# Products of values and scores written as two column tiles of 64 tokens

## Chip, cores and metric

The kernel runs on one core of one Trainium2 chip. The metric is the device time of one execution in microseconds (us); lower is better. Of the kernel before there are three timed executions and one profiled execution.

## What is computed

Three layers in a row: a linear recurrence with a decaying state per head, a feed-forward layer of width 2048 with a clipped square as its nonlinearity, and a gated feed-forward layer of width 1536. In the reference, cut to what matters here:

```python
batch, n_heads, seq, head_dim = (4, 8, 768, 48)          # all float32
for t in range(S):                                        # recurrence
    cur = np.einsum('bhd,bhe->bhde', u[None] * kt, vt)
    y[:, :, t] = np.einsum('bhd,bhde->bhe', rt, state + cur)
    state = wt[:, :, :, None] * state + np.einsum('bhd,bhe->bhde', kt, vt)
x = y as 3072 tokens x 384
h = x @ w_in;  g = where(h >= 1, h, where(h <= -1, 0, (h + 1)**2 / 4));  x = g @ w_out
g = x @ w_gate; x = (g * sigmoid(g) * (x @ w_val)) @ w_out
```

## The kernel before

The 3072 tokens are worked on in 8 "halves" g of 384 tokens, and each half in 3 windows w of 128 tokens. A channel-major operand lies with one head on partitions 0 to 47 and the other head of a pair on 64 to 111, so there are 4 pairs of heads.

The recurrence is done in windowed form. For each window TensorE does a list of "fills", each into a PSUM bank that VectorE or ScalarE then empties ("drains"):

- KT (L1082): 4 transposes of the scaled keys.
- AT, two fills in one (L1089): the scores of keys against receptances, a matmul with 48 rows for each head. The two heads of a pair lie on partitions 0 to 47 and 64 to 111. VectorE copies the part above the diagonal into the SBUF tiles `att0` and `att1`, 4 heads each (L894).
- ST (L1098): 4 products of the key transposes (128 x 112) with 96 columns of values: what the window adds to the state.
- Y: the output of the window, 128 tokens (partitions) x 384 channels, one bank. First, unless the state is still zero, 4 matmuls of the receptances with the decayed state (L1104, 128 tokens on the stationary side, 96 moving columns). Then, for each of the 8 heads, one matmul that adds the scores times the values (L1108): stationary operand `att[h % 2][:, h // 2, :]`, 128 x 128; moving operand 48 columns of `vn`. VectorE adds the diagonal term (L908), which gives `x_by_token`.
- XT (L1113): 3 transposes of `x_by_token`, from which ScalarE and VectorE make the high and low parts of x (L681, L911).

These products are plain fp32. For each the trace holds two LDWEIGHTS and two MATMUL records; such a pair of one LDWEIGHTS and one MATMUL is called a record pair below. So L1108 has 16 in a Y fill and 384 in all, in 24 Y fills. The large products of the feed-forward layers (L1039 for the way in, L1063 for the way out) are written as three fp32r products of high and low parts, each with a 128 x 128 stationary operand and 384 moving columns, and leave one record pair each.

The order is written out by hand. The fills of half 0 stand at the head of the program, before the first feed-forward product; that head also loads and splits the weights of layer 1. After that `phase1` runs 8 halves of 16 slots. A slot j has on TensorE the 9 products of `tile_in` (j + 2), then the fills of the next half that `WIN_SLOTS` gives to the slot, then the 9 products of `tile_out` (j):

```python
    FILLS = [("KT", 0, 0), ("AT", 0, 0), ("AT", 0, 1), ("ST", 0, 0), ("KT", 1, 0), ("Y", 0, 0),
             ("AT", 1, 0), ("AT", 1, 1), ("XT", 0, 0), ("ST", 1, 0), ("KT", 2, 0), ("Y", 1, 0),
             ("AT", 2, 0), ("AT", 2, 1), ("XT", 1, 0), ("ST", 2, 0), ("Y", 2, 0), ("XT", 2, 0)]
    WIN_SLOTS = {3 + i: (2 * i, 2 * i + 1) for i in range(NF // 2)}
    WIN_SLOTS[11], WIN_SLOTS[12] = (NF - 2,), (NF - 1,)
```

So the Y fills of halves 1 to 7, 21 of them, stand in slots 5, 8 and 11 of the half before, each between other matmuls of TensorE. `phase2`, the gated layer, has no fills. TensorE takes its instructions in program order; waits on semaphores guard the banks (`bank_free`) and the operands: a Y fill waits for the decayed state (`st_dec`) and for both score tiles (`at_out`), and its last matmul increments `fill`, for which the drain L908 waits.

Of the kernel before, what the change touches and what calls it, by code (L numbers as in the profile page):

```python
# [31 lines left out]
B, H, S, D = 4, 8, 768, 48  # L32
# [3 lines left out]
WIN = 128  # L36
# [47 lines left out]
def build_program(nc, w_d, kd_d, rd_d, rn_d, kn_d, vn_d, u_d, cst_d, w1i_d, w1o_d, w2g_d, w2v_d,  # L84
                  w2o_d, rs_d, ks_d, vs_d, ws_d, us_d, out_d, x2_d, ys_d):
    ctx = ExitStack()
    with ctx:
        at = [nc.sbuf_base + (-nc.sbuf_base) % 32]

        def place(name, shape, dt, offset=None):  # L90

            size = 2 if dt == mybir.dt.bfloat16 else 4
            for n in shape[1:]:
                size *= n
            if offset is None:
                offset = at[0]
                at[0] += (size + 31) // 32 * 32
            assert offset + size <= nc.sbuf_usable_end, (name, offset + size)
            return nc.alloc_sbuf_tensor_at(name, shape, dt, offset=offset), offset + size
# [36 lines left out]
        vn, _ = place("v_by_token", [P, NW, DM], F32)  # L136
        uu, _ = place("u_rows", [P, DM], F32)
        att = [place(f"att{i}", [P, 4, WIN], F32)[0] for i in range(2)]
# [14 lines left out]
        for n in ("hi", "lo"):  # L153
            t, o = place(f"w2gv_a{n}", [P, NA, 2, KT * P], F32R, o)
# [3 lines left out]
        for n in ("hi", "lo"):  # L158
            t, o = place(f"w2gv_b{n}", [P, J2 - NA, 2, KT * P], F32R, o)
            w2b.append(t)  # L160
        w2o = []
        for n in ("hi", "lo"):
            t, o = place(f"w2o{n}", [P, J2, DM], F32R, o)
# [55 lines left out]
        def state_pairs(w, parity):  # L219

            return 1 if parity == 1 and w == NW - 1 else NPAIR
# [26 lines left out]
        def bank_of(g, f):  # L248

            return (attb + hid + acc)[f % 8] if isinstance(g, int) and g == 0 else attb[f % NBANK]  # L250

        def cols(w):
            return slice(w * WIN, (w + 1) * WIN)
# [776 lines left out]
        def _(e):  # L1030
# [36 lines left out]
            def do_fill(g, f, parity):  # L1067
                kind, w, n = FILLS[f]
                if kind == "AT" and n == 1:
                    return  # L1070
                out = bank_of(g, f)
                bank_free(g, f)
                if kind == "KT":
                    first_half = isinstance(g, int) and g == 0
                    if w == 0 and not first_half:
                        e.wait_ge(scaled, (g + 1) * (2 * NPAIR))
                    if w == 0 and isinstance(g, int) and g == 0:
                        e.wait_ge(ld["cst"], 16)
                    for p in range(NPAIR):
                        if w == 0 and first_half:  # L1080
                            e.wait_ge(scaled, 2 * p + 2)
                        m = e.transpose(out[:, p * PR:(p + 1) * PR], kd[:, p, cols(w)], ident[0:PR, 0:PR])  # L1082
                elif kind == "AT":
                    other = bank_of(g, f + 1)
                    bank_free(g, f + 1)
                    for p in range(NPAIR):
                        for i, o in enumerate((out, other)):
                            r = slice(64 * i, 64 * i + D)
                            m = e.matmul(o[:, p * WIN:(p + 1) * WIN], kd[r, p, cols(w)], rd[r, p, cols(w)],  # L1089
                                         start=True, stop=True)  # L1090
                            if p == NPAIR - 1 and i == 0:
                                m.then_inc(fill, 1)
                elif kind == "ST":
                    e.wait_ge(kt_out, g * NW + (w + 1))
                    if w == 0:
                        e.wait_ge(ld["vn"], (g + 1) * 16)
                    for p in range(state_pairs(w, parity)):
                        m = e.matmul(out[0:PR, p * 2 * D:(p + 1) * 2 * D], ktk[w % 2][:, p * PR:(p + 1) * PR],  # L1098
                                     vn[:, w, p * 2 * D:(p + 1) * 2 * D], start=True, stop=True)
                elif kind == "Y":  # L1100
                    e.wait_ge(st_dec, g * NW + (w + 1))
                    row_start = w == 0 and parity == 0
                    for p in range(0 if row_start else NPAIR):
                        e.matmul(out[:, p * 2 * D:(p + 1) * 2 * D], rd[:, p, cols(w)], sbar[:, p, :],  # L1104
                                 start=(p == 0), stop=False, skip_group_check=True)
                    e.wait_ge(at_out, g * (2 * NW) + (2 * w + 2))
                    for h in range(H):
                        m = e.matmul(out[:, h * D:(h + 1) * D], att[h % 2][:, h // 2, :], vn[:, w, h * D:(h + 1) * D],  # L1108
                                     start=(row_start and h == 0), stop=(h == H - 1), skip_group_check=True)
                elif kind == "XT":  # L1110
                    e.wait_ge(y_out, g * NW + (w + 1))
                    for k in range(KT):
                        m = e.transpose(out[:, k * P:(k + 1) * P], xn[:, w, k * P:(k + 1) * P], ident)  # L1113
                m.then_inc(fill, 1)

            def bank_free(g, f):

                n_bank = 8 if isinstance(g, int) and g == 0 else NBANK
                gg, ff = (g, f - n_bank) if f >= n_bank else (g - 1, f - n_bank + NF)
                if isinstance(gg, int) and gg < 0:  # L1120
                    return
                kind, w, n = FILLS[ff]
                if kind == "KT":
                    e.wait_ge(kt_out, gg * NW + (w + 1))
                elif kind == "AT":
                    e.wait_ge(at_out, gg * (2 * NW) + (2 * w + n + 1))
                elif kind == "ST":
                    e.wait_ge(st_out, gg * (2 * NW) + (2 * w + 2))
                elif kind == "Y":
                    e.wait_ge(y_out, gg * NW + (w + 1))  # L1130
                else:
                    e.wait_ge(xl_out, gg * NW + (w + 1))
# [3 lines left out]
            for f in range(NF):  # L1136
                do_fill(0, f, 0)
# [19 lines left out]
            def slot(g, j, parity, next_half, after_next):  # L1157
                last = isinstance(g, int) and g == NG - 1
                if j + 2 < J1:
                    tile_in(g, j + 2, parity)  # L1160
                elif not last:
                    tile_in(g + 1, j + 2 - J1, 1 - parity)
                else:
                    tile_in2(0, j + 2 - J1, 0)
                if last and j == 4:
                    e.wait_ge(w_sum, NG + 2)
                    e.matmul(attb[2][0:1, 0:1], bad[:, OPS_CHECK:OPS_CHECK + 1], ones[:, :], start=True, stop=True).then_inc(w_tot, 1)
                if next_half:
                    for f in WIN_SLOTS.get(j, ()):
                        do_fill(g + 1, f, 1 - parity)  # L1170
                tile_out(1, g, j, w1o)
# [76 lines left out]
```

## Time and profile before

| | us |
|---|---|
| median of 3 executions | 1050.95 |
| lowest, highest | 1050.66, 1052.82 |
| profiled execution, its own time | 1050.49 |
| its span, first to last instruction | 1048.6 |
| TensorE matmuls busy | 1004.0 (96%) |
| TensorE weight loads busy | 990.1 (94%) |
| VectorE busy | 555.8 (53%) |
| ScalarE busy | 394.5 (38%) |
| GpSimd busy | 133.6 (13%) |

"Busy" is the share of the span in which an engine had a record open. A MATMUL record is longer than the time for which it keeps the next one away, since matmuls are pipelined; what one costs a full TensorE is seen from the distance between starts. PE is the matmul side of TensorE, PEld its weight loads. The profiled execution is 1.9 us longer than its span, and 0.46 us below the median of the three.

### The profile page before, as it was taken

The page shows a single profiled execution, that of the slowest core. Times are in us where ns is not written, and L with a number is a line of the kernel's source. Part 1 is how long each engine was busy: PE and PEld are TensorE (multiplying, and loading weights), DVE is VectorE, ACT ScalarE, POOL GpSimd, SP SyncE. Part 2 cuts the span into 40 slices and gives each one's busy share as a digit, 9 for nine tenths or more (in the row PEclk, how much of TensorE's full clock was granted, in tenths as well). Part 3 has the DMA queues.
Part 4 walks back from the last instruction along what each step waited for, and adds up shares of the span by engine and source line. Part 5 has one row for each costly group of instructions (what it writes and reads, how often), then busy time and mean ns, then how long its engine had stood idle before and what let it go on. Part 6 is the DMA issues. An engine that isn't in the chain of part 4 may idle for free.

```text
span 1048.6 us, 15818 instructions
## 1 busy us (share of the span) xinstructions
PE 1004.0 (96%) x6162; PEld 990.1 (94%) x6162; DVE 555.8 (53%) x958; ACT 394.5 (38%) x799; POOL 133.6 (13%) x90
## 2 busy tenths in 40 slices
PE   1689999999999999999999999999999999999997
PEld 0679999999999999999999999999999999999997
DVE  7866584774947759477444443343434343433332
ACT  3445344453454535544366532222222222222221
POOL 4650030110301203002026320000000000000000
PEclk9989999999999999999999999999999999999999
DMA  6450140400503105030033211001010101010000
GB/s 225 149 181 27 30 142 1 144 27 3 168 1 132 39 2 170 1 121 24 1 121 98 91 53 46 2 1 46 1 45 0 45 0 45 0 45 0 23 1 25
DMA packets 23199, 59.63 MB, mean 57 GB/s; under 512 B 2657, under 2 KB 11489, under 8 KB 23137
## 3 DMA queue, kind: packets, MB, share of 16 engines
q1 hardware_dynamic: 23136, 58.79, 17.1%
q8 instruction: 41, 0.67, 0.3%
q14 instruction: 22, 0.17, 0.1%
HBM read 49.34 MB, written 9.44 MB: 56 GB/s over the span
## 4 chain that ended last, share of the span: by engine, by line
PE 92%; DVE 4%; issue 1%; ACT 1%; DMA 1%; SPq 0%; DVEq 0%; ACTq 0%
PE bank L1039 47%; PE bank L1063 34%; PE bank L1108 4%; PE bank L1089 2%; PE bank L1104 2%; PE bank L1098 1%; PE bank L1082 1%; PE bank L1113 1%; DVE w_window L835 1%; DVE r_by_channel L860 1%; DVE k_by_channel L852 1%; DVE suf L830 1%; DVE w_by_channel L843 0%; DMA w_by_channel<-in_w_channel 0%; DMA ring<-in_w_out 0%
## 5 line engine op out<-in xcount | busy, mean ns | idle before, releaser
L690 ACT ACTIVATE ghi<-gate 128x384 fp32r<-128x384 f32 x224 | 117.9, 526 | 256.7 <-PE bank L1063 111.3
L916 DVE TENSOR_TENSOR glo<-gate,ghi 128x384 fp32r<-128x384 f32 x224 | 136.5, 610 | 115.8 <-ACT ghi L690 113.4
L933 DVE TENSOR_TENSOR gate<-bank,gate 128x384 f32<-128x384 f32 x96 | 53.6, 558 | 221.6 <-ACT gate L794 221.6
L1039 PE MATMUL bank<-xlo,w2gv_ahi 128*128 128x384 f32 x480 | 162.1, 338 | 0.0
L1039 PE MATMUL bank<-xhi,w2gv_alo 128*128 128x384 f32 x480 | 162.1, 338 | 0.0
L1039 PE MATMUL bank<-xhi,w2gv_ahi 128*128 128x384 f32 x480 | 162.1, 338 | 0.0
L1063 PE MATMUL bank<-ghi,w1ohi 128*128 128x384 f32 x384 | 136.9, 357 | 3.1 <-DVE glo L916 3.1
L794 ACT ACTIVATE gate<-bank 128x384 f32<-128x384 f32 x96 | 47.3, 493 | 234.1 <-PE bank L1039 234.1
L1039 PE MATMUL bank<-xhi,w1ihi 128*128 128x384 f32 x384 | 130.7, 340 | 1.3 <-DVE xlo L911 1.3
L1039 PE MATMUL bank<-xlo,w1ihi 128*128 128x384 f32 x384 | 130.5, 340 | 0.0
L1039 PE MATMUL bank<-xhi,w1ilo 128*128 128x384 f32 x384 | 130.4, 339 | 0.0
L1063 PE MATMUL bank<-glo,w1ohi 128*128 128x384 f32 x384 | 129.7, 338 | 0.0
L1063 PE MATMUL bank<-ghi,w1olo 128*128 128x384 f32 x384 | 129.6, 338 | 0.0
L923 DVE SCALAR_TENSOR_TENSOR gate<-bank,gate 128x384 f32<-128x384 f32 x128 | 70.9, 554 | 106.5 <-ACT gate L699 106.3
L697 ACT ACTIVATE gate<-bank 128x384 f32<-128x384 f32 x128 | 62.7, 490 | 101.2 <-PE bank L1039 101.2
L1063 PE MATMUL bank<-ghi,w2ohi 128*128 128x384 f32 x288 | 97.3, 338 | 0.0
L1063 PE MATMUL bank<-ghi,w2olo 128*128 128x384 f32 x288 | 97.3, 338 | 0.0
L1063 PE MATMUL bank<-glo,w2ohi 128*128 128x384 f32 x288 | 97.3, 338 | 0.0
L1039 PEld LDWEIGHTS bank<-xhi,w2gv_alo 128*128 128x128 f32 x480 | 90.1, 188 | 0.0
L1039 PEld LDWEIGHTS bank<-xlo,w2gv_ahi 128*128 128x128 f32 x480 | 90.1, 188 | 0.0
L1039 PEld LDWEIGHTS bank<-xhi,w2gv_ahi 128*128 128x128 f32 x480 | 90.1, 188 | 0.0
L1063 PEld LDWEIGHTS bank<-ghi,w1ohi 128*128 128x128 f32 x384 | 72.2, 188 | 7.4 <-DVE glo L916 4.8
(81 smaller groups left out, 1607.9 us busy)
## 6 DMA issues: line engine op xcount, KB each, us to landing
w_by_channel<-in_w_channel SPq DMA_DIRECT2D x16, 339.5 KB, 3.8
k_by_channel<-in_k_channel SPq DMA_DIRECT2D x16, 336.0 KB, 4.8
r_by_channel<-in_r_channel SPq DMA_DIRECT2D x16, 336.0 KB, 5.5
ring<-in_w_out SPq DMA_DIRECT2D x28, 192.0 KB, 2.7
r_k_diag<-in_r_token SPq DMA_DIRECT2D x8, 576.0 KB, 7.0
k_by_token<-in_k_token SPq DMA_DIRECT2D x8, 576.0 KB, 8.0
v_by_token<-in_v_token SPq DMA_DIRECT2D x8, 576.0 KB, 9.1
x_t<-ring SPq DMA_DIRECT2D x8, 576.0 KB, 3.3
```

The costliest lines, as they stand in the source:

```text
L690: e.activation(ghi[j % 2][:, :], gate[j % 2][:, :], ACT.Copy).then_inc(M["hi", ph], 1)
L697: e.activation(q, hid[j % 2][:, 0:T], ACT.Relu, bias=0.5, scale=0.5).then_inc(M["q", 1], 1)
L794: e.activation(gate[j % 2][:, :], hid[j % 2][:, 0:T], ACT.Sigmoid).then_inc(M["q", 2], 1)
L830: e.tensor_tensor_scan(suf[:, p, ::-1], w_at[:, p, :0:-1], last_of_window[0:PR, ::-1], 0.0, ALU.mult, ALU.add).then_inc(scan, 1)
L916: e.tensor_tensor(glo[j % 2][:, :], gate[j % 2][:, :], ghi[j % 2][:, :].bitcast(F32), ALU.subtract)\
L923: e.scalar_tensor_tensor(q, hid[j % 2][:, 0:T], 1.0, q, ALU.max, ALU.min).then_inc(M["g", 1], 1)
L933: e.tensor_tensor(q, hid[j % 2][:, 0:T], q, ALU.mult).then_inc(M["t", 2], 1)
L1039: m = e.matmul(out, w_of(a, k), x_of(b_, k), start=start and i == 0, stop=stop and i == total - 1)
L1063: m = e.matmul(acc[k][:, 0:T], wo[a][:, j, k * P:(k + 1) * P], gs[b_][:, :], start=(j == 0 and i == 0), stop=(j == J[ph] - 1 and i == 2))
L1089: m = e.matmul(o[:, p * WIN:(p + 1) * WIN], kd[r, p, cols(w)], rd[r, p, cols(w)], start=True, stop=True)
L1104: e.matmul(out[:, p * 2 * D:(p + 1) * 2 * D], rd[:, p, cols(w)], sbar[:, p, :], start=(p == 0), stop=False, skip_group_check=True)
L1108: m = e.matmul(out[:, h * D:(h + 1) * D], att[h % 2][:, h // 2, :], vn[:, w, h * D:(h + 1) * D], start=(row_start and h == 0), stop=(h == ...
```

## The change

Each of the 8 matmuls of a Y fill at L1108 becomes two. The stationary operand of one is the first 64 columns (tokens) of the score tile, that of the other the last 64, and the results go to PSUM partitions 0 to 63 and 64 to 127 of the same bank and the same columns. The moving operand, 48 columns of values, is the same for both. All 128 rows are contracted in each. The waits, the increment at the end, the other fills and the drain stay as they are.

```diff
                     e.wait_ge(at_out, g * (2 * NW) + (2 * w + 2))
                     for h in range(H):
-                        m = e.matmul(out[:, h * D:(h + 1) * D], att[h % 2][:, h // 2, :], vn[:, w, h * D:(h + 1) * D],
-                                     start=(row_start and h == 0), stop=(h == H - 1), skip_group_check=True)
+                        for t in (slice(0, WIN // 2), slice(WIN // 2, WIN)):
+                            m = e.matmul(out[t, h * D:(h + 1) * D], att[h % 2][:, h // 2, t],
+                                         vn[:, w, h * D:(h + 1) * D], start=(row_start and h == 0),
+                                         stop=(h == H - 1), skip_group_check=True)
```

A Y fill then has 16 such matmuls, 32 record pairs, instead of 8 and 16.

## Rows read from the trace of the kernel before

**Rows 1.** The page: busy totals, and the chain that ended last, by engine.

```profile
PE 1004.0 (96%) x6162; PEld 990.1 (94%) x6162; DVE 555.8 (53%) x958; ACT 394.5 (38%) x799; POOL 133.6 (13%) x90
PE 92%; DVE 4%; issue 1%; ACT 1%; DMA 1%; SPq 0%; DVEq 0%; ACTq 0%
```

**Rows 2.** Stretches: start:end length, then busy us (records) by engine, clock, DMA.

```profile
45.00:57.40 12.40, 10.54 (x55) 10.01 (x56) 10.72 (x18) 5.42 (x12) 6.69 (x6) 1.00 0.63 190
60.80:67.60 6.80, 4.91 (x16) 4.57 (x17) 1.11 (x3) 1.36 (x4) 1.70 (x2) 0.50 0.63 186
80.00:552.00 472.00, 471.78 (x3159) 461.87 (x3157) 303.61 (x546) 221.36 (x454) 59.47 (x26) 1.00 0.20 64
```

**Rows 3.** Groups of TensorE in 80 to 552 us: busy us, mean ns, idle before.

```profile
L1063 PE MATMUL bank<-ghi,w1ohi 128*128 128x384 f32 x342 | 122.6, 359 | 3.1 <-DVE glo L916 3.1
...
L1108 PE MATMUL bank<-v_by_token,att 128*128 128x48 f32 x336 | 40.1, 272 | 0.0
```

**Rows 4.** Timeline of the weight loads around a Y fill: start us, us.

```profile
173.03 0.97 PEld L1104 LDWEIGHTS bank<-state_decayed,r_by_channel 112*128 112x128 f32 x8
173.92 1.87 PEld L1108 LDWEIGHTS bank<-v_by_token,att 128*128 128x128 f32 x16
175.71 0.19 PEld L1063 LDWEIGHTS bank<-ghi,w1ohi 128*128 128x128 f32 x1
```

**Rows 5.** The same around an ST fill, whose stationary operand has 112 columns.

```profile
168.68 0.87 PEld L1098 LDWEIGHTS bank<-v_by_token,k_token 128*112 128x112 f32 x8
169.47 0.19 PEld L1063 LDWEIGHTS bank<-ghi,w1ohi 128*128 128x128 f32 x1
```

**Rows 6.** Timeline of the matmuls around an AT fill.

```profile
163.66 0.34 PE L1039 MATMUL bank<-xlo,w1ihi 128*128 128x384 f32 x1
163.83 0.33 PE L1039 MATMUL bank<-xhi,w1ilo 128*128 128x384 f32 x1
164.09 1.16 PE L1089 MATMUL bank<-r_by_channel,k_by_channel 48*128 48x128 f32 x16
165.19 0.44 PE L1063 MATMUL bank<-ghi,w1ohi 128*128 128x384 f32 x1
165.47 0.34 PE L1063 MATMUL bank<-glo,w1ohi 128*128 128x384 f32 x1
```

**Rows 7.** The weight loads of that AT fill.

```profile
164.09 0.97 PEld L1089 LDWEIGHTS bank<-r_by_channel,k_by_channel 48*128 48x128 f32 x16 [0.24 <-issue]
```

**Rows 8.** The matmuls around the check of the weights' sum, one stationary column.

```profile
552.00 0.34 PE L1039 MATMUL bank<-xhi,w1ilo 128*128 128x384 f32 x1
552.27 0.19 PE L1167 MATMUL bank<-ones,w_bad 112*1 112x1 f32 x2
552.38 0.44 PE L1063 MATMUL bank<-ghi,w1ohi 128*128 128x384 f32 x1
552.67 0.34 PE L1063 MATMUL bank<-glo,w1ohi 128*128 128x384 f32 x1
```

**Rows 9.** L1167's matmuls by themselves: duration ns min/median/max.

```profile
L1167 PE MATMUL bank<-ones,w_bad x2: 163/164/164, 552.3 to 552.3; 112*1 112x1 f32 x2
```

**Rows 10.** TensorE in the head of the program: the three Y fills of half 0.

```profile
29.13 3.58 PE L1108 MATMUL bank<-v_by_token,att 128*128 128x48 f32 x16
...
48.85 3.65 PE L1108 MATMUL bank<-v_by_token,att 128*128 128x48 f32 x16 [1.44 <-DVE att L894]
...
57.89 1.91 PE L1108 MATMUL bank<-v_by_token,att 128*128 128x48 f32 x16
```

**Rows 11.** VectorE in the head: the drains of these fills, with the wait before.

```profile
40.21 0.56 DVE L908 TENSOR_TENSOR x_by_token<-bank,r_k_diag 128x384 f32<-128x384 f32 x1
...
52.54 0.56 DVE L908 TENSOR_TENSOR x_by_token<-bank,r_k_diag 128x384 f32<-128x384 f32 x1 [1.45 <-PE bank L1108]
...
60.72 0.56 DVE L908 TENSOR_TENSOR x_by_token<-bank,r_k_diag 128x384 f32<-128x384 f32 x1
```

**Rows 12.** VectorE before and after a Y fill of the steady part.

```profile
157.90 0.56 DVE L916 TENSOR_TENSOR glo<-gate,ghi 128x384 fp32r<-128x384 f32 x1
...
160.98 0.56 DVE L908 TENSOR_TENSOR x_by_token<-bank,r_k_diag 128x384 f32<-128x384 f32 x1 [0.48 <-PE bank L1108]
```

## The prediction

> **What bounds the kernel.** I read the page's totals first: TensorE's matmul side is open for 96% of the span and holds 92% of the chain that ended last [rows 1]. An average over stages says nothing of one fill, so the next view is the table of stretches: from 80 to 552 us, which holds 21 of the 24 Y fills, TensorE is busy for 471.78 of 472.00 us, VectorE for 303.61 and ScalarE for 221.36 [rows 2]. The only wait of its matmuls there is 3.1 us for `glo`, before the first slots have settled, and L1108 itself waits for nothing [rows 3]. So a microsecond that TensorE no longer needs in this stretch shortens the run by a microsecond, unless a new wait takes it. The last view is TensorE's timeline around the fills, where the reader should look at the distance between starts and not at the length of records.
>
> **What a Y fill costs now.** The 16 loads of L1108 start at 173.92 and the next load starts at 175.71: 1.79 us, 0.112 for a record pair [rows 4]. What sets the 0.112? Not the 48 moving columns: L1104 moves 96, and its 8 loads take 173.92 - 173.03 = 0.89 us, 0.111 each [rows 4]. With a stationary operand of 112 columns it is less, (169.47 - 168.68) / 8 = 0.099 [rows 5]. So these products are bound by the loading of weights, and its time goes with the number of stationary columns: 0.112 x 112/128 = 0.098 agrees. Nothing of the fill is hidden: the last L1108 load is followed at its usual distance by the load of L1063.
>
> **What the change makes of it.** It removes 16 record pairs with 128 stationary columns and adds 32 with 64. No wait, DMA, queue entry or drain moves. There are three terms.
>
> 1. One load of 64 columns. In proportion, 0.112 / 2 = 0.056 us. On a straight line through the two rows (0.013 less for 16 columns less) it is 0.112 - 4 x 0.013 = 0.060. The work of the matmul is shorter: the fp32r products start every (552.00 - 551.65) / 2 us, or 0.175, for 384 columns (the rows at 163.66 and 163.83 show one step [rows 6]), so two passes over 48 columns are 0.175 x 96/384 = 0.044. I take 0.056, with 0.060 as the upper end. For the lower end: the two matmuls of L1167, with one stationary column, last 0.164 each and 0.19 together, so they start 0.026 apart [rows 8, 9].
>
> 2. Whether the two halves run side by side. The trace has no tile of 64 columns. The nearest row is the AT fill, two tiles that share the array by rows. Its 16 loads take 0.97 us in all [rows 7]; with the last one some 0.19 long their starts spread over 0.78 us, where 15 steps of 0.112 would be 1.68. They start in pairs: 7 steps from pair to pair of 0.112 are 0.78. So two tiles that don't overlap in the array load and multiply at the same time, with the full rate each. The halves of the change alternate between their tiles in the same way as the heads do at L1089. If columns behave as rows do, 32 record pairs cost 16 x 0.056 = 0.896 us; if not, 32 x 0.056 = 1.79 us, all that is spent today. I take the first, because the one row with two tiles shows it; both ends stay in the range.
>
> 3. Going into the other shape of tile and back. The AT fill shows the price. Without a fill, the matmul after the one at 163.83 would start at 164.005; the one at 165.47 is the second of L1063, so the first effectively began at 165.295. The fill occupied 1.29 us, and 8 pairs at 0.112 explain 0.90, which leaves 0.39 [rows 6]. L1167, whose operand has 112 rows and one column, thus a tile narrow in columns, shows the same: from 552.175 to 552.67 - 0.175 = 552.495 is 0.32 us, of which its two matmuls explain 0.05: 0.27 are left [rows 8]. At L1104 beside L1108, both with 128 columns, there is no such gap [rows 4]. The new Y fill is in between: its first load that nothing covers is half as long as that of AT. I take 0.33, with 0.27 and 0.39 as ends.
>
> The Trainium skill, "TensorEngine Tiling (Array Packing)", section "Tiling Modes", says that a change of mode drains the engine, and that tiles load and multiply in parallel. The rows above agree with both, for tiles by rows; no row shows the second for columns. The page "TensorE: Matmul & The Clock Gate" gives about 62 ns for a MATMUL in one of its two ways of decoding; that speaks against this change, for 32 of them would be 1.98 us, and the run would be 1062 by it. The 16 at L1089 start in 0.89 us, less than 62 ns each, but a queue filled beforehand could feed such a short burst.
>
> The new fill: 0.896 + 0.33 = 1.23 us against 1.79, a saving of 0.56. Over 21 fills that is 11.8 us. By the ends: (1.79 - 0.96 - 0.39) x 21 = 9.2 and (1.79 - 0.83 - 0.27) x 21 = 14.5.
>
> Does it reach the end? The drain L908 waits for TensorE already (0.48 us at 160.98) and starts earlier. After the fill TensorE needs `glo`, ready at 158.46, 2.3 us before its load at 160.74 or so; the new fill leaves 1.7 us of that [rows 12]. What is late next in these slots is again TensorE. VectorE and ScalarE have 36% and 53% of the stretch free.
>
> **Half 0, in the head.** Here TensorE is not the bound. The first Y fill ends before 33 us and its drain runs at 40.21 without a wait for it; the drain of the third, at 60.72, waits for nothing either [rows 10, 11]. Only the second is on the path: its 16 record pairs last 3.65 us, twice the steady distance, and the drain at 52.54 waited 1.45 us for it. It would take 16 x 0.112 = 1.8 us and some drain, so VectorE's own order of work takes over as soon as 1.45 us are gained. What follows (the last weights, ScalarE's copies) may take part back: I take 1.0 us, with 0 and 1.45 as ends. There is a side cost. From 60.8 to 67.6 us the granted clock is 0.50, the level of 1.2 GHz, after a pause of TensorE [rows 2]. Less work before that moves the stretch or lengthens it; some 13 feed-forward matmuls stood in it at about 0.32 us and not 0.175, so I allow 2 us either way.
>
> **The sum**, on the profiled execution: 1050.5 - 11.8 - 1.0 = 1037.7. The median of the three was 0.46 above it, which gives 1038.1.
>
> **Rivals.**
>
> *One tile at a time (0.18).* The loads of the halves follow each other, because both read all 128 partitions where the heads of AT read different ones, or TensorE starts no more than one record pair each 0.056 us, the mean of the AT fill. Both give the same price: 32 x 0.056 + 0.33 = 2.12 us, 0.33 more than now, 6.9 us in all, nothing gained in the head: 1058. Slower. It decides wherever two column tiles start more than (1.79 - 0.33) / 16 = 0.091 us apart from pair to pair. For it: no row shows two column tiles, or more than 16 record pairs at this rate. Against it: L1089, and the 0.026 between the two of L1167.
>
> *Side by side, but load and matmul of a tile one after the other (0.04).* 0.056 + 0.044 = 0.100 for a pair of tiles, 16 x 0.100 + 0.33 = 1.93: 0.14 more, 3 us over 21 fills: 1054. Against it: in L1089 the load and the matmul of 2 x 128 columns fit into one 0.112.
>
> *The burst outruns what feeds it (0.07).* About half of the 32 come at 0.028, the rest slower, at 0.05: 0.45 + 0.80 + 0.33 = 1.58, a saving of 0.21, with the head 5.4 us: 1045.5.
>
> *Gained and given back (0.04).* A later wait, for the weights or for `glo`, eats it: 1050.5. The free 1.7 us after each fill speak against it.
>
> That the first half, at partition 0, is not made a narrow tile, with a change of shape at every matmul (16 x 0.3 us more in a fill, about 100 us in all), I give 0.01.
>
> **How the numbers follow.** The forecast has 0.66, with its own range from 1034 to 1042. A measurement of this kernel tells about 0.2%, 2.1 us, from no change. Faster: 0.66 + 0.07 = 0.73. Within: the give-back and the lower edge of the 0.100 case, 0.06. Slower: 0.18, most of the 0.04, 0.01: 0.21 after rounding. The range goes from 1034.5 up to 1056, which takes in the milder part of the one-at-a-time case.
>
> **What the changed profile would show.** Right: 768 record pairs at L1108; loads that start in pairs some 5 ns apart, with 0.056 us to the next pair; from the first L1108 matmul of a steady fill to the first of L1063 about 1.1 to 1.2 us; the other fills unchanged; L908's wait for L1108 shorter; the drain of the second Y fill of the head some 1.4 us earlier. Wrong: loads at even steps of 0.056, or pairs more than 0.09 apart; gaps inside the fill; a wait for `glo` that was not there. The overhead is wrong if the gap before the first load and after the last matmul together isn't 0.27 to 0.39 us.

## The result, and the profile after

The changed kernel takes 1039.11 us (median of 4, 1037.70 to 1040.16) where the kernel before takes 1051.38 (median of 4): 12.3 us less, ratio 0.9881, 95% interval 0.9864 to 0.9898. The forecast was 1038.1, with a range from 1034.5 to 1056. On another occasion the changed kernel took 1039.31 us and the kernel before 1051.24, ratio 0.9883 (0.9864 to 0.9902).

The page after, totals and chain, to be read against [rows 1]:

```profile
PE 989.0 (95%) x6546; PEld 971.8 (94%) x6546; DVE 555.3 (53%) x958; ACT 394.4 (38%) x799; POOL 135.2 (13%) x90
PE 92%; DVE 3%; issue 2%; DMA 1%; ACT 1%; SPq 0%; DVEq 0%; ACTq 0%
```

There are 384 record pairs more (6546 for 6162) and yet TensorE's matmul side is open for 15 us less. It still holds 92% of the chain. VectorE, ScalarE and GpSimd have as many instructions as before, and are busy for the same time within 2 us.

The weight loads around a Y fill, and then its matmuls (start us, us), to be read against [rows 4]:

```profile
174.27 1.01 PEld L1109 LDWEIGHTS bank<-v_by_token,att 128*64 128x64 f32 x32
175.34 0.19 PEld L1063 LDWEIGHTS bank<-ghi,w1ohi 128*128 128x128 f32 x1
```

```profile
173.95 0.39 PE L1104 MATMUL bank<-state_decayed,r_by_channel 112*128 112x96 f32 x2
174.27 1.14 PE L1109 MATMUL bank<-v_by_token,att 128*64 128x48 f32 x32
175.34 0.44 PE L1063 MATMUL bank<-ghi,w1ohi 128*128 128x384 f32 x1
```

From the first L1109 load to the load of L1063 it is 1.07 us, where it was 1.79. Within the fill the loads start at 0, 7, 55, 62, 111, 118, 169, 176, 228, 234 ns and so on: two loads 7 ns apart, and about 58 ns to the next pair. Now there are gaps ahead of the fill and behind it. The whole price of a fill is reckoned as in the third term of the prediction: from where the next fp32r matmul would have started to where the first one effectively did. For L1104 and L1108 together that was 2.68 us before and is 2.13 after. L1104 takes 0.89 of both, so L1108 went from 1.79 to 1.24. In this trace 18 fills saved 0.55 each and the three without L1104 0.53, 11.5 us in all.

Groups of TensorE in the steady stretch, to be read against [rows 3]:

```profile
L1063 PE MATMUL bank<-ghi,w1ohi 128*128 128x384 f32 x339 | 121.9, 360 | 0.1
...
L1109 PE MATMUL bank<-v_by_token,att 128*64 128x48 f32 x672 | 23.9, 224 | 0.0
```

The only wait left in that line is 0.1 us, and no new one has come up in this stretch. The stretches (start:end length, busy us by engine, clock, DMA), to be read against [rows 2]:

```profile
34.30:54.80 20.50, 11.34 (x84) 10.49 (x84) 20.00 (x29) 8.76 (x19) 13.69 (x12) 0.50 0.42 127
...
61.58:68.40 6.82, 5.82 (x18) 5.85 (x19) 1.53 (x4) 1.80 (x4) 0.28 (x1) 0.50 0.92 244
...
78.65:85.48 6.83, 5.79 (x18) 5.79 (x19) 5.98 (x12) 1.95 (x4) 1.23 (x1) 0.50 0.33 93
...
85.48:541.00 455.52, 455.38 (x3468) 442.21 (x3467) 296.01 (x535) 218.23 (x448) 57.99 (x25) 1.00 0.20 65
```

The granted clock is 0.50, the level of 1.2 GHz, in three of them. The first holds the second Y fill of the head, and explains why it takes twice the time that it would take at the full clock. In the trace before, the clock column reads 1.00 there [rows 2], but the matmuls contradict it: the AT fill behind that Y fill takes 2.08 us in both traces, where one in the steady part takes 1.16 [rows 6].

```profile
52.44 2.08 PE L1089 MATMUL bank<-r_by_channel,k_by_channel 48*128 48x128 f32 x16
```

The second, at 61.58, is the stretch that the kernel before had too. The third is one that the trace before lacks: TensorE had paused before it for `glo`, and 18 matmuls then started 0.32 us apart and not 0.175.

The head, TensorE and then VectorE, to be read against [rows 10, 11]:

```profile
28.95 1.95 PE L1109 MATMUL bank<-v_by_token,att 128*64 128x48 f32 x32
...
48.55 1.95 PE L1109 MATMUL bank<-v_by_token,att 128*64 128x48 f32 x32 [1.43 <-DVE att L894]
...
55.66 1.14 PE L1109 MATMUL bank<-v_by_token,att 128*64 128x48 f32 x32
```

```profile
39.90 0.56 DVE L908 TENSOR_TENSOR x_by_token<-bank,r_k_diag 128x384 f32<-128x384 f32 x1
...
51.44 0.56 DVE L908 TENSOR_TENSOR x_by_token<-bank,r_k_diag 128x384 f32<-128x384 f32 x1
...
60.09 0.56 DVE L908 TENSOR_TENSOR x_by_token<-bank,r_k_diag 128x384 f32<-128x384 f32 x1
```

The second Y fill is 1.7 us shorter and its drain no longer waits. The drain starts 1.1 us earlier, of which 0.3 is that this execution was ahead there already. So 0.8 us is gained at this point, and not the whole wait of 1.45: now VectorE's own work before the drain ends last.

### The profile page after: what moved, and what is told of

It reads as the page before. It is cut to its first block, busy times and chain, and to the rows that moved or that the text cites. A ratio compares the mean times of both kernels' runs of the same rounds, so it can differ in the third digit from the quotient of the medians.

```text
span 1038.3 us, 16586 instructions
## 1 busy us (share of the span) xinstructions
PE 989.0 (95%) x6546; PEld 971.8 (94%) x6546; DVE 555.3 (53%) x958; ACT 394.4 (38%) x799; POOL 135.2 (13%) x90
## 4 chain that ended last, share of the span: by engine, by line
PE 92%; DVE 3%; issue 2%; DMA 1%; ACT 1%; SPq 0%; DVEq 0%; ACTq 0%
PE bank L1039 48%; PE bank L1063 35%; PE bank L1089 2%; PE bank L1109 2%; PE bank L1104 2%; PE bank L1098 1%; PE bank L1082 1%; PE bank L1115 1%; DVE k_by_channel L852 1%; DMA ring<-in_w_out 1%; DVE w_by_channel L843 1%; ACT w_checked L669 1%; DVE r_by_channel L860 0%; DVE suf L830 0%; DMA w_by_channel<-in_w_channel 0%
## 5 line engine op out<-in xcount | busy, mean ns | idle before, releaser
L1063 PE MATMUL bank<-ghi,w1ohi 128*128 128x384 f32 x384 | 137.9, 359 | 3.3 <-DVE glo L916 3.2
L1063 PE MATMUL bank<-glo,w1ohi 128*128 128x384 f32 x384 | 130.4, 340 | 0.0
L1063 PE MATMUL bank<-ghi,w1olo 128*128 128x384 f32 x384 | 130.2, 339 | 0.0
L1063 PE MATMUL bank<-glo,w2ohi 128*128 128x384 f32 x288 | 97.9, 340 | 0.0
L1063 PE MATMUL bank<-ghi,w2ohi 128*128 128x384 f32 x288 | 97.1, 337 | 0.0
L1063 PE MATMUL bank<-ghi,w2olo 128*128 128x384 f32 x288 | 97.1, 337 | 0.0
L1063 PEld LDWEIGHTS bank<-ghi,w1ohi 128*128 128x128 f32 x384 | 72.5, 189 | 8.7 <-DVE glo L916 5.0
```

What stands on the lines that cost most here:

```text
L1063: m = e.matmul(acc[k][:, 0:T], wo[a][:, j, k * P:(k + 1) * P], gs[b_][:, :], start=(j == 0 and i == 0), stop=(j == J[ph] - 1 and i == 2))
```

## The experiments

Each is an edit of the changed kernel. The ratio compares a kernel with the kernel before as it ran beside it, whose median was 1051.1 to 1052.0 us. "Fill" is the price of L1104 and L1108 together, reckoned as above, in each kernel's trace.

| kernel | median us | ratio to before (95%) | fill us |
|---|---|---|---|
| before | 1051 to 1052 | 1 | 2.68 |
| changed | 1039.1 | 0.9881 (0.9864 to 0.9898) | 2.13 |
| lower halves first, then upper | 1051.2 | 1.0002 (0.9989 to 1.0015) | 2.87 |
| the same by four heads | 1048.0, one run | | 2.48 |
| the same by two heads | 1042.2, one run | | 2.17 |
| even heads split only | 1065.1 | 1.0129 (1.0109 to 1.0148) | 3.35 |
| four tiles of 32 | 1035.2 | 0.9849 (0.9830 to 0.9867) | 1.88 |
| L1104 in two tiles too | 1037.6 | 0.9864 (0.9841 to 0.9887) | 1.93 |
| four tiles, both | 1032.1 | 0.9826 (0.9807 to 0.9844) | 1.68 |
| ST fill in two tiles too | 1044.3 | 0.9945 (0.9929 to 0.9962) | 2.13 |
| steady fills only | 1039.5 | 0.9890 (0.9872 to 0.9909) | 2.13 |
| half 0 only | 1051.5 | 1.0008 (0.9996 to 1.0020) | 2.68 |

### Is it the two tiles side by side? Lower halves first

```diff
-                    for h in range(H):
-                        for t in (slice(0, WIN // 2), slice(WIN // 2, WIN)):
+                    for t in (slice(0, WIN // 2), slice(WIN // 2, WIN)):
+                        for h in range(H):
```

> The same 16 matmuls of a Y fill, in another order: first the lower halves of all 8 heads, then the upper halves. Theory (side by side only where neighbours in program order lie in different tiles): the 16 record pairs of one tile follow each other at 0.058 us, so a fill is 32 x 0.058 + 0.30 = 2.16 us and not 1.24; over 21 fills 19 us more than the changed kernel, about 1058, slower than before. Rival (each tile is fed by itself, whatever the order): starts in pairs as now, 1039.

The same instructions in another order give the whole gain back. The weight loads of one fill (start us, us):

```profile
174.30 1.75 PEld L1109 LDWEIGHTS bank<-v_by_token,att 128*64 128x64 f32 x32
176.10 0.19 PEld L1063 LDWEIGHTS bank<-ghi,w1ohi 128*128 128x128 f32 x1
```

1.80 us from load to load. So half as many stationary columns are worth nothing by themselves; what shortens the fill is that two tiles work at once. But the fill, 2.87 - 0.89 = 1.98 us, is 0.18 us shorter than expected. The starts show why. A record doesn't name its tile, but the 32 starts fall into two even chains of 16, with steps of 58 ns: one from 0 to 869 ns, which I take for the lower tile, and one from 741 ns on, for the upper. The first of the upper chain starts when three of the lower ones (752, 811, 869 ns) are still to come. TensorE does look ahead past a busy tile, by three record pairs here. Both theories were too simple. In total the run was also some 7 us better than the 1058 expected: 4 of them are the 0.18 in 21 fills, the rest I can't place. By the fills alone it should be 4 us slower than the kernel before; measured is no difference, with an interval that ends at 1.6 us more.

### How far it looks ahead: groups of two and of four heads

```diff
-                    for h in range(H):
-                        for t in (slice(0, WIN // 2), slice(WIN // 2, WIN)):
+                    for h0 in range(0, H, 2):              # and 4
+                        for t in (slice(0, WIN // 2), slice(WIN // 2, WIN)):
+                            for h in (h0, h0 + 1):         # range(h0, h0 + 4)
```

> The matmuls of a Y fill in groups of two heads: the lower halves of two heads, then their upper halves. In the kernel with all lower halves first, the first upper record pair started when two of the lower ones had not yet begun. Theory (TensorE looks two record pairs past those that wait for a busy tile): each group of four record pairs starts while the last two of the group before run, so both tiles stay fed; a fill costs 0.12 us more than in the changed kernel at most, from its first and last group alone. Rival (overlap ends where neighbours share a tile, apart from the seam between groups): some 0.058 x 2 lost at each of 8 groups, 0.5 to 0.9 us more.

> The same in groups of four heads, eight record pairs of one tile in a row. Theory (two record pairs of look-ahead): a group starts 6 steps of 0.058 after the one before it, 4 groups take 3 x 0.35 + 0.47 = 1.52 us and not 0.94, so a fill costs 0.58 us more than in the changed kernel, a little more than before the change. Rival (look-ahead of four or more): 0.23 more.

The loads of a fill by twos:

```profile
175.70 1.05 PEld L1110 LDWEIGHTS bank<-v_by_token,att 128*64 128x64 f32 x32
176.80 0.19 PEld L1063 LDWEIGHTS bank<-ghi,w1ohi 128*128 128x128 f32 x1
```

and by fours:

```profile
175.04 1.36 PEld L1110 LDWEIGHTS bank<-v_by_token,att 128*64 128x64 f32 x32
176.46 0.19 PEld L1063 LDWEIGHTS bank<-ghi,w1ohi 128*128 128x128 f32 x1
```

By twos, four record pairs of one tile in a row, a fill costs 0.04 us more than in the changed kernel: the rival (0.5 to 0.9) is out, and the theory's limit of 0.12 held. By fours it costs 0.35 more. That is neither the 0.58 of a look-ahead of two nor the 0.23 of four. The second chain of loads starts at 274 ns, with three of the first (286, 344, 402 ns) to come, as in the kernel with all lower halves first; each later group of this fill starts 274 ns after the one before it. By twos, too, each upper group starts with three loads of the lower group before it to come. Three record pairs fit all three kernels. Each of these two kernels was run only once, so the argument rests on the traces: 1042.2 us is 3 more than the changed kernel, of which the fills explain 21 x 0.04 = 0.8.

### The price of changing the shape of tiles: even heads only

```diff
-                        for t in (slice(0, WIN // 2), slice(WIN // 2, WIN)):
+                        for t in ((slice(0, WIN // 2), slice(WIN // 2, WIN)) if h % 2 == 0 else (slice(0, WIN),)):
```

> Only the even heads are split in two column tiles; the odd heads keep one matmul of 128 columns. Theory (each way into the narrow shape and back costs 0.30 us): 8 x 0.058 + 8 x 0.112 + 4 x 0.30 = 2.56 us for a fill, 1.32 more than the changed kernel, over 21 fills 28 us: 1067, slower than before. Rival (the 0.30 is paid only beside the fp32r products or with a wait, not at each change of shape): 8 x 0.058 + 8 x 0.112 + 0.30 = 1.66, 9 us more than the changed kernel: 1048.

```profile
177.95 2.48 PE L1109 MATMUL bank<-v_by_token,att 128*64 128x48 f32 x24
180.25 0.42 PE L1063 MATMUL bank<-ghi,w1ohi 128*128 128x384 f32 x1
```

The fill costs 3.35 - 0.89 = 2.46 us. Its record pairs explain 8 x 0.058 + 8 x 0.112 = 1.36, so the four ways in and out cost 1.10, 0.27 each. The theory (2.56 us) held, the rival's 1.66 did not. The price is paid at each change of shape, without any wait in between, and it turns the gain of 12 us into a loss of 13 (1065.13 against 1051.95). 0.27 is the lower end that the one-column product gave [rows 8]; in the changed kernel it is 1.24 - 16 x 0.058 = 0.31.

### Narrower still: four tiles of 32

```diff
-                        for t in (slice(0, WIN // 2), slice(WIN // 2, WIN)):
+                        for t in [slice(i * 32, i * 32 + 32) for i in range(4)]:
```

> Four column tiles of 32 tokens each and not two of 64; 64 record pairs in a Y fill. Theory (a tile's load goes with its columns, 0.029 us for 32, then the two passes of 48 columns bound it at 0.044 to 0.047): 16 steps of 0.047 + 0.30 = 1.05 us for a fill against 1.24 now, 0.19 x 21 = 4 us less than the changed kernel: 1035. Rival (TensorE can't start record pairs faster than the 0.029 apart of now): 64 x 0.029 + 0.30 = 2.16, 1058.

```profile
172.34 0.75 PEld L1109 LDWEIGHTS bank<-v_by_token,att 128*32 128x32 f32 x64
173.16 0.19 PEld L1063 LDWEIGHTS bank<-ghi,w1ohi 128*128 128x128 f32 x1
```

64 record pairs in less time than 32: four loads 7 ns apart, and 43 ns to the next four, which is two passes of 48 moving columns (0.044) and no longer a load. The time, 1035.2, is the expected 1035, but the fill saved 0.25 us and not the expected 0.19. The row rules out a limit of 0.029 us on the start of record pairs: here they start every 0.011 on average. The Trainium skill, "TensorE: Matmul & The Clock Gate", "Back-to-back issue gap", gives a floor of some 25 ns for small matmuls, and 62 where they are decoded the slower way. The floor of 25 ns may hold within one tile; for matmuls in different tiles these runs show 7 ns between starts.

### L1104 in column tiles too

```diff
-                        e.matmul(out[:, p * 2 * D:(p + 1) * 2 * D], rd[:, p, cols(w)], sbar[:, p, :],
-                                 start=(p == 0), stop=False, skip_group_check=True)
+                        for t in (slice(0, WIN // 2), slice(WIN // 2, WIN)):
+                            e.matmul(out[t, p * 2 * D:(p + 1) * 2 * D], rd[:, p, cols(w)][:, t], sbar[:, p, :],
+                                     start=(p == 0), stop=False, skip_group_check=True)
```

> The products with the decayed state (L1104, 96 moving columns) written as two column tiles as well, so that the change of tile shape stands before them and is paid once for both. Theory (the longer of load and matmul bounds a tile: 0.058 against two passes of 96 columns, 0.088): 8 steps of 0.09 = 0.72 us and not 8 x 0.111 = 0.89, 0.17 x 18 = 3 us less than the changed kernel: 1036. Rival (loads bound alone, 0.058): 0.47, 7.6 us less: 1031.5. Rival (load and matmul of a tile don't overlap, 0.058 + 0.088 = 0.146): 1.17, 5 us more: 1044.

```profile
172.98 0.69 PEld L1105 LDWEIGHTS bank<-state_decayed,r_by_channel 112*64 112x64 f32 x16
173.61 1.04 PEld L1110 LDWEIGHTS bank<-v_by_token,att 128*64 128x64 f32 x32
```

In the middle of the first row, pairs start every 82 ns, near the expected 88 for two passes of 96 columns and far from a load's 58. The two lines of products follow each other without a gap, so the way in is paid once. Both rivals (0.058 and 0.146 us a step) are out. A fill takes 1.93 and not 2.13 us, 3.6 us over 18 fills. The time, 1037.6, is 1.5 us below the changed kernel, whose interval it overlaps; that this edit by itself is a gain is shown by the trace and not by the times.

### The two together

Four tiles for L1104 and L1108 both.

> Four column tiles of 32 tokens for the products with the decayed state and for those of scores and values alike, one change of shape before both. Theory (a tile's steps are the two passes of the moving columns: 8 x 0.083 and 16 x 0.043): 0.66 + 0.69 + 0.30 = 1.65 us for both against 2.13 in the changed kernel and 1.88 with four tiles at L1108 alone: 21 x 0.25 + 18 x 0.23 = 9.4 us less than the changed kernel, about 1030. Rival (the gains don't add, because TensorE runs out of prepared record pairs in a burst of 96): 1035 as with four tiles at L1108 alone, or more.

```profile
169.25 0.87 PE L1105 MATMUL bank<-state_decayed,r_by_channel 112*32 112x96 f32 x32
169.93 0.87 PE L1110 MATMUL bank<-v_by_token,att 128*32 128x48 f32 x64
170.73 0.45 PE L1063 MATMUL bank<-ghi,w1ohi 128*128 128x384 f32 x1
```

96 record pairs in 1.48 us, and a fill of 1.68 us. It is the fastest version, 1032.1 us, 7 us below the changed kernel beside it (1039.31). Both lines together were expected at 1.65 us, so the gains add, and the rival is out. The time is 2 us above the expected 1030; the fills account for 0.5 of them, the rest lies outside.

### Where it doesn't pay: the ST fill

```diff
-                        m = e.matmul(out[0:PR, p * 2 * D:(p + 1) * 2 * D], ktk[w % 2][:, p * PR:(p + 1) * PR],
-                                     vn[:, w, p * 2 * D:(p + 1) * 2 * D], start=True, stop=True)
+                        for a, b in ((0, 64), (64, PR)):
+                            m = e.matmul(out[a:b, p * 2 * D:(p + 1) * 2 * D], ktk[w % 2][:, p * PR + a:p * PR + b],
+                                         vn[:, w, p * 2 * D:(p + 1) * 2 * D], start=True, stop=True)
```

> The changed kernel with the ST fill (L1098) as two column tiles as well, 64 and 48 columns, 96 moving columns, 8 record pairs of 0.099 us before. Theory (a burst must save more than the 0.30 of the change of shape): 8 steps of 0.083 + 0.30 = 0.96 us and not 0.80, so 21 x 0.16 = 3.4 us more than the changed kernel, 1042.5. Rival (the narrower tile wins wherever a load bounds): 21 x 0.13 = 2.7 us less, 1036.5.

```profile
168.44 0.87 PE L1099 MATMUL bank<-v_by_token,k_token 128*64 128x96 f32 x16
```

The fill went from 0.80 to 1.00 us, and four of the 21 ST fills, which hold only one product, by 0.30: 17 x 0.20 + 4 x 0.30 = 4.6 us. The times say 5 to 6. The theory's direction and size held, the rival's gain did not come. Eight record pairs of 0.099, with 96 moving columns, save 0.13 and cost one change of shape; a fill of two record pairs pays the change of shape and saves nothing.

### Steady fills or head

The split is done only where `g != 0`, or only where `g == 0`.

> Column tiles only in the 21 Y fills of halves 1 to 7; half 0 in the head keeps the matmuls of 128 columns. Theory (the steady fills make the change: 0.55 us each by the trace of the changed kernel): 21 x 0.55 = 11.5 us less than before, ratio 0.989, and the same as the changed kernel within 1 us. Rival (a part of the 12.3 us comes from the head): a smaller gain, by as much as the head-only kernel gains.

> Column tiles only in the three Y fills of half 0. Theory (the second fill's drain starts some 1 us earlier, and the clock in the head may take it back): between 1 us less and 2 us more than before; ratio 0.999 to 1.002. Rival (the head's savings count in full, three fills of 1.7, 1.7 and 0.6 us): 4 us less, ratio 0.996.

> The changed kernel once more, beside the others on the same chip. Theory: 1039 within 1 us, ratio 0.988. Some of its executions have a second stretch at the half clock after the head, others not, so their times spread over 2 to 3 us. Rival (the first comparison was off): another ratio.

The steady fills alone give 0.9890, the whole change 0.9883 beside it; the head alone gives 1.0008 (0.9996 to 1.0020). So the gain comes from the 21 steady fills, and none from the head that these runs can tell. The rival of 4 us is out.

## Why the prediction was right

**The bound.** TensorE stayed the bound of the stretch, without a new wait. (Of the 3.1 us of waiting that the prediction read into it, 2.9 end at 79.64 us and lie ahead of it, as a row below shows.) The gain per fill arrives one for one: 21 fills at 0.55 are 11.5 us, and the kernel with steady fills only gained 11.8 (1051.24 - 1039.46).

**Term 1, a load of 64 columns.** Taken 0.056, upper end 0.060; measured 0.058. The straight line through the 112- and 128-column rows was as near as the proportion. 16 x 0.002 is 0.03 us in a fill.

**Term 2, side by side.** Right, and now shown for columns: by the starts 7 ns apart, and by the order alone, which costs the whole gain. The prediction carried this over from two tiles that share the array by rows. It noted that the halves alternate between their tiles as the heads do at L1089; that this is a condition, within three record pairs, is what the groups of heads show.

**Term 3, the change of shape.** Taken 0.33 with ends 0.27 and 0.39; it is 0.31 here and 0.27 between heads.

The fill came out at 1.24 us and not 1.23, by errors of terms 1 and 3 that cancel, and the forecast saving of 11.8 us stands against 11.5.

**The rivals.** One tile at a time needed steps of 0.056 us from load to load, or more than 0.091 from pair to pair; the trace has 0.007 and 0.058. Load and matmul one after the other needed 0.100. The burst that outruns what feeds it needed slower steps in its second half; the loads keep the same step up to the last, at 876 ns. A narrow first half that is not made one would have cost a change of shape at every matmul; the even-heads kernel shows what that is like. The 62 ns for each MATMUL, which the prediction weighed against the change, did not show either: the 32 of this fill start every 0.029 us on average.

**The head.** This term, 1.0 us, is the one that failed: the kernel with column tiles in the head alone is 0.3 us slower than before, and its interval allows a gain of 0.4 at most. The prediction took the second Y fill alone to be on the path. Its wait did go, but the 0.8 us gained there meets another wait some 6 us later. The next time that VectorE makes the low part of x, it waits for ScalarE's high part. Before, and then after:

```profile
58.18 0.56 DVE L911 TENSOR_TENSOR xlo<-bank,xhi 128x384 fp32r<-128x384 f32 x1 [0.84 <-ACT xhi L681]
```

```profile
57.56 0.56 DVE L911 TENSOR_TENSOR xlo<-bank,xhi 128x384 fp32r<-128x384 f32 x1 [1.58 <-ACT xhi L681]
```

This wait grew by 0.74 us. ScalarE copies weights of layer 1 before that instruction, and in the trace after it waits 1.13 us for the DMA of one of them, until 56.13. That the arrival of the weights takes the gain back is read from the traces; the prediction had named these weights and copies as what might. No run took this wait away.

TensorE before, at its first feed-forward product and at the wait in the third slot:

```profile
63.56 0.66 PE L1039 MATMUL bank<-xhi,w1ihi 128*128 128x384 f32 x1 [1.26 <-DVE xlo L911]
...
79.64 0.44 PE L1063 MATMUL bank<-ghi,w1ohi 128*128 128x384 f32 x1 [2.90 <-DVE glo L916]
```

after:

```profile
62.58 0.66 PE L1039 MATMUL bank<-xhi,w1ihi 128*128 128x384 f32 x1 [1.26 <-DVE xlo L911]
...
79.69 0.69 PE L1063 MATMUL bank<-ghi,w1ohi 128*128 128x384 f32 x1 [3.18 <-DVE glo L916]
```

and in the steady-only kernel, whose head is that of before:

```profile
62.69 0.66 PE L1039 MATMUL bank<-xhi,w1ihi 128*128 128x384 f32 x1 [1.26 <-DVE xlo L911]
```

So the 1.0 us by which the first feed-forward product starts earlier in the trace after is not shown to come from the change: it starts 0.9 earlier with the old head too, and in a second trace of the changed kernel it starts at 63.81. The products of the third slot start at 79.6 both before and after. TensorE waits there for `glo`, and `glo` for VectorE's scaling of the next half. The same stretch of VectorE and of GpSimd, before:

```profile
72.55 2.71 DVE L852 TENSOR_TENSOR k_by_channel<-k_by_channel,suf 112x384 f32<-112x384 f32 x1
75.18 3.00 DVE L860 TENSOR_TENSOR r_by_channel<-r_by_channel,w_by_channel 112x384 f32<-112x384 f32 x1
78.10 0.55 DVE L852 TENSOR_TENSOR k_by_channel<-k_by_channel,suf 112x384 f32<-112x384 f32 x1
```

```profile
72.15 2.69 POOL L618 TENSOR_TENSOR r_k_diag<-r_k_diag,k_by_token 128x1152 f32<-128x1152 f32 x1 [9.65 <-DMA k_by_token<-in_k_token]
74.92 2.85 POOL L622 TENSOR_TENSOR r_k_diag<-r_k_diag,u_rows 128x1152 f32<-128x1152 f32 x1
```

Two instructions of the scaling take 2.7 and 3.0 us where the next one of the same form takes 0.55, and just while GpSimd makes its two diagonal products, whose start was set by a DMA. In the trace after GpSimd's products start 0.4 us later, and again two instructions of the scaling take 3.0 us. That the two engines get in each other's way is read from traces alone; no run took it away. That the head gains nothing was run.

**The side cost of the clock.** It was given 2 us either way. In the profiled execution the stretch at 1.2 GHz from 78.65 us costs 18 matmuls x 0.145 = 2.6 us: the fills of half 1 begin at 85.56, where it was 82.90. The span still fell by 10.3, since 13.0 was gained after that point: 11.5 in the fills, and about 1.4 because the some 4800 fp32r matmuls behind it start 0.3 ns closer together on average (175.65 ns and not 175.94). The kernels of the experiments fall on either of these two values without a pattern that I can see. The steady-only trace, whose head is that of before, has a half-clock stretch there too (mean clock 0.79 from 78 to 86 us), after a shorter pause of 2.68 us, where the kernel before paused for 2.90 without one; so the stretch can't be laid to the change. It costs 1.3 us in that trace, and is likely one reason why executions of one kernel spread by 2 to 4 us.

**Luck in the number.** The forecast saving of 12.8 us and the measured 12.3 are closer than the terms: the fills gave 11.5, the head nothing that could be told, and the 0.8 that remains lies within the spread of the executions.

## What to carry to other kernels

Where short fp32 products follow each other and the distance between their starts goes with the stationary columns, cutting these columns into tiles that write different partitions lets the loads run at the same time, down to what the moving columns cost in their two passes; the order must alternate between tiles within about three record pairs. Each way into another tile shape and back costs about 0.3 us, so put all products of one shape in a row and convert a burst only if it saves more than that: 16 record pairs that took 1.79 us were worth it, 8 that took 0.80 were not. A microsecond saved in a stage whose end is set by something else, here most likely by weights that arrive by DMA, is worth nothing, even if the next step starts earlier. And where one execution starts a step 1 us earlier, look at a second one before the change gets the credit.

## What was not expected of the hardware

Four column tiles start record pairs 7 ns apart, every 0.011 us on average over 64 of them at L1108, and 96 with those of L1104 take 1.48 us. And a tile's work starts ahead of earlier instructions for another, busy tile: in the kernel with the lower halves first the first upper load starts 11 ns before the fourteenth lower one, if the two chains of starts are the two tiles, and the matmuls' starts in the trace form two overlapping chains in the same way. So "in program order", as the kernel was described above, holds within a tile. The Trainium skill, "TensorE: Matmul & The Clock Gate", "The mechanism", says that loads may be pulled ahead but matmuls start in strict order; these traces agree with the first part and not with the second, as far as starts that the profiler gives can tell.
